# Fused attention, routed experts and mixer: the weighing of two heads in two column halves, and the seam before the mixer

## What is computed

```python
# attention, for each batch and head
q_d, k_d, v_d = means over groups of 4 positions          # 144 positions
out_up    = repeat(softmax(q_d @ k_d.T / 8) @ v_d, 4)
out_local = softmax(mask(q @ k.T / 8)) @ v                # mask: |i - j| < 4
x = out_up + out_local
# experts: one of 8 per position (w1: 512 x 1024, w2: 1024 x 512)
y[b, s] = p[e] * (relu(x[b, s] @ w1[e]) @ w2[e])
# mixer
u   = y + (relu(y.T @ w_tok1) @ w_tok2).T
out = u + relu(u @ w_ch1) @ w_ch2
```

## Time and profile before

| | us |
|---|---|
| median of 3 runs | 924.77 (924.2 to 925.93) |
| the profiled execution, own time | 922.74 |
| its span, as the trace has it | 921.1 |
| mean granted TensorE clock in it | 0.981 of full |

### The profile page before, as it was taken

How to read it: one execution, slowest core, us unless ns; L and a number is a source line. 1 busy time by engine, 2 the same in 40 slices (tenths; PEclk the granted TensorE clock), 3 DMA queues, 4 the chain that set the end, 5 groups by cost and what they waited for, 6 DMA issues and landing times.

```text
span 921.1 us, 13441 instructions
## 1 busy us (share of the span) xinstructions
PE 866.1 (94%) x4511; PEld 719.9 (78%) x4512; DVE 441.6 (48%) x893; ACT 348.8 (38%) x876; POOL 233.2 (25%) x355
## 2 busy tenths in 40 slices
PE   6888989889899999999999959999999999999998
PEld 4676767657478888888878847999999889999997
DVE  5786978878663462435663547312122353121211
ACT  4666775655253352435562433111111121111110
POOL 6886876774322212221212210000000000000000
PEclk9899999999799999999999989999999999999999
DMA  9558776630162842346652532002010010000000
GB/s 160 110 101 204 152 140 139 148 129 12 52 214 73 281 167 94 119 148 219 211 181 79 194 95 99 1 1 69 1 55 15 7 62 1 1 35 1 35 1 35
DMA packets 94128, 88.44 MB, mean 96 GB/s; under 512 B 63213, under 2 KB 68991, under 8 KB 94079
## 3 DMA queue, kind: packets, MB, share of 16 engines
q1 hardware_dynamic: 90203, 75.21, 29.8%
q0 software_dynamic: 3840, 12.59, 4.1%
q10 hardware_dynamic: 36, 0.01, 0.0%
HBM read 72.31 MB, written 15.48 MB: 95 GB/s over the span
## 4 chain that ended last, share of the span: by engine, by line
PE 75%; DVE 8%; POOL 7%; issue 4%; DMA 3%; ACT 2%; SPq 1%; POOLq 0%; ACTq 0%; DVEq 0%
PE bank L1648 16%; PE bank L1650 16%; PE bank L1649 16%; PE bank L1700 4%; PE bank L1707 4%; PE bank L1701 4%; PE bank L1691 2%; POOL asb L735 2%; PE bank L1525 2%; DMA stage<-in_moe_w 1%; PE bank L1478 1%; PE bank L1572 1%; PE bank L1656 1%; DVE aT L1121 1%; POOL ptmp L721 1%
## 5 line engine op out<-in xcount | busy, mean ns | idle before, releaser
L1371 DVE SCALAR_TENSOR_TENSOR h2l<-bank,h2h 128x384 fp32r<-128x384 f32 x72 | 40.1, 558 | 190.0 <-ACT h2h L1022 190.0
L1022 ACT ACTIVATE h2h<-bank 128x384 fp32r<-128x384 f32 x72 | 35.4, 492 | 229.7 <-PE bank L1650 229.7
L1648 PE MATMUL bank<-uTh,W 128*128 128x384 f32 x288 | 98.1, 340 | 0.0
L1649 PE MATMUL bank<-uTl,W 128*128 128x384 f32 x288 | 97.5, 338 | 0.0
L1650 PE MATMUL bank<-uTh,W 128*128 128x384 f32 x288 | 97.1, 337 | 0.0
L1650 PE MATMUL bank<-W,h2l 128*128 128x512 f32 x216 | 84.5, 391 | 0.0
L1648 PE MATMUL bank<-W,h2h 128*128 128x512 f32 x216 | 84.3, 390 | 0.0
L1649 PE MATMUL bank<-W,h2h 128*128 128x512 f32 x216 | 84.1, 389 | 0.0
L1309 DVE TENSOR_TENSOR W<-stage,W 128x1024 fp32r<-128x1024 f32 x56 | 66.7, 1220 | 21.2 <-ACT W L968 18.7
L1700 PE MATMUL bank<-W,hTh 128*128 128x512 f32 x184 | 76.3, 415 | 0.0
L968 ACT ACTIVATE W<-stage 128x1024 fp32r<-128x1024 f32 x56 | 58.0, 1055 | 45.2 <-DVE ysb L1327 24.3
(11 more groups left out here) (224 smaller groups left out, 1804.6 us busy)
## 6 DMA issues: line engine op xcount, KB each, us to landing
stage<-in_moe_w SPq DMA_DIRECT2D x56, 512.0 KB, 4.6
vl<-in_v SPq DMA_DIRECT2D x40, 128.0 KB, 3.7
qraw<-in_q SPq DMA_DIRECT2D x32, 144.0 KB, 4.9
kraw<-in_k SPq DMA_DIRECT2D x32, 144.0 KB, 5.3
v<-in_v SPq DMA_DIRECT2D x8, 576.0 KB
ub<-y_dr SPq DMA_DIRECT2D x18, 256.0 KB, 4.5
out<-ob SPq DMA_DIRECT2D x18, 256.0 KB, 2.1
x_dr<-xrow SPq DMA_DIRECT2D x16, 256.0 KB, 3.3
```

Of the source, the lines that this page charges most:

```text
L1022: act.activation(dst, bank[bk][:, 0:width], ACT.Relu).then_inc(relu_hi, 1)
L1371: dve.scalar_tensor_tensor(dst, bank[bk][:, 0:width], 0.0, hi.bitcast(F32), ALU.max, ALU.subtract).then_inc(bank_free, 1)
L1648: pe.matmul(ps, ah, bh, start=first, stop=False)
L1649: pe.matmul(ps, ah, bl, start=False, stop=False)
```

## The change

It has two parts.

1. `weigh` issues a pair's two heads as two matmuls, each with a stationary operand of 64 columns and the probabilities of one head alone. The first writes partitions 0 to 63 of the bank, the second 64 to 127, over the same columns. So the sums of a unit lie on 128 partitions in half as many columns, and `attended` takes them in one DVE instruction in place of two. `scores` is left as it is.
2. At the seam, the scaling in place (L1381), its wait and its semaphore go. `u_rows` reads the unscaled tile and multiplies by the share as it adds. PE gets `keep_busy(36, bank[3])` after the transpose L1740, ahead of its wait for `moe_done`.

```diff
             def attended(n):
                 if u < NDS:
                     pr, j = u // NPQ, u % NPQ
-                    for h in range(2):
-                        rows = slice(h * D, (h + 1) * D)
-                        last = dve.tensor_scalar_mul(odT[rows, hb % 2, pr, j * PQ:(j + 1) * PQ],
-                                                     ps_o[n % 2][rows, h * PQ:(h + 1) * PQ], 1.0 / POOLF)
+                    dve.tensor_scalar_mul(odT[:, hb % 2, pr, j * PQ:(j + 1) * PQ], ps_o[n % 2][:, 0:PQ], 1.0 / POOLF
+                                          ).then_inc(x_done, 1)
                 else:
...
-                    for h in range(2):
-                        rows = slice(h * D, (h + 1) * D)
-                        o = ps_o[n % 2][rows, 0:4 * lq].rearrange("d (r h n f) -> d r h n f", r=HP, h=2, f=POOLF)
-                        x = xT[rows, hb % 2 * HP:hb % 2 * HP + HP, Q0[t]:Q0[t] + lq].rearrange(
-                            "d r (n f) -> d r n f", f=POOLF)
-                        up = odT[rows, hb % 2, :, Q0[t] // POOLF:Q0[t] // POOLF + n4]
-                        last = dve.tensor_tensor(x, o[:, :, h], bc(up.unsqueeze(3), [D, HP, n4, POOLF]), ALU.add)
-                last.then_inc(x_done, 1)
+                    o = ps_o[n % 2][:, 0:HP * lq].rearrange("d (r n f) -> d r n f", r=HP, f=POOLF)
+                    x = xT[:, hb % 2 * HP:hb % 2 * HP + HP, Q0[t]:Q0[t] + lq].rearrange("d r (n f) -> d r n f", f=POOLF)
+                    up = odT[:, hb % 2, :, Q0[t] // POOLF:Q0[t] // POOLF + n4]
+                    dve.tensor_tensor(x, o, bc(up.unsqueeze(3), [P, HP, n4, POOLF]), ALU.add).then_inc(x_done, 1)
...
             def x_lo_tile(pr, i):
                 dve.scalar_tensor_tensor(xl[:, cols], ub[:, i, :], share, xh[:, cols].bitcast(F32), ALU.mult,
                                          ALU.subtract).then_inc(xl_done, 1)
-                dve.wait_ge(xl_done, 9 * pr + i + 1)
-                dve.tensor_scalar_mul(ub[:, i, :], ub[:, i, :], share).then_inc(xf_done, 1)
...
             def u_rows(pr, hb):
-                dve.wait_ge(xf_done, 9 * pr + (9 if hb else NK5))
+                dve.wait_ge(xl_done, 9 * pr + (9 if hb else NK5))
...
-                    tt(ub[rows, i, :], bank[2 + kk][rows, :], ub[rows, i, :], ALU.add).then_inc(bank_free, 1)
+                    dve.scalar_tensor_tensor(ub[rows, i, :], ub[rows, i, :], prob[rows, 9 * pr + i:9 * pr + i + 1],
+                                             bank[2 + kk][rows, :], ALU.mult, ALU.add).then_inc(bank_free, 1)
...
             def weigh(n):
+                heads = [slice(h * D, (h + 1) * D) for h in range(2)]
...
                     for kt in range(NPQ):
-                        mm = pe.matmul(ps_o[n % 2][:, 0:2 * PQ], vd[:, hb % 2, kt, pr * P:(pr + 1) * P],
-                                       aT[0:PQ, n % 2, kt * 2 * PQ:(kt + 1) * 2 * PQ], start=(kt == 0),
-                                       stop=(kt == NPQ - 1))
+                        for h in range(2):
+                            c = pr * P + h * D
+                            mm = pe.matmul(ps_o[n % 2][heads[h], 0:PQ], vd[:, hb % 2, kt, c:c + D],
+                                           aT[0:PQ, n % 2, (2 * kt + h) * PQ:(2 * kt + h + 1) * PQ], start=(kt == 0),
+                                           stop=(kt == NPQ - 1))
...
                     for pr in range(HP):
-                        cols = slice(pr * 2 * lq, (pr + 1) * 2 * lq)
-                        mm = pe.matmul(ps_o[n % 2][:, cols], vl[:, hb % 2, t, pr * P:(pr + 1) * P],
-                                       aT[:, n % 2, cols], start=True, stop=True)
+                        for h in range(2):
+                            c = pr * P + h * D
+                            mm = pe.matmul(ps_o[n % 2][heads[h], pr * lq:(pr + 1) * lq], vl[:, hb % 2, t, c:c + D],
+                                           aT[:, n % 2, (HP * pr + h) * lq:(HP * pr + h + 1) * lq], start=True, stop=True)
...
             pe.transpose(bank[7][:, 0:NT], probT[:, :], ident[0:NT, 0:NT]).then_inc(prob_turned, 1)
+            keep_busy(36, bank[3])
             pe.wait_ge(moe_done, 1)
```

More of the change, by code:

```diff
@@ L446, in build @@
         xh_done, xl_done = sem("xh_done"), sem("xl_done")
-        xf_done = sem("xf_done")
         bank_full = sem("bank_full")
```

## The result

The change takes **920.10 us** (median of 5 runs, 916.91 to 922.08) against 924.77 (5 runs, 923.34 to 925.93): a ratio of 0.9947, 95% interval 0.9922 to 0.9971. Predicted were 916.6 with a range of 911.5 to 922.5. So 4.7 us of an expected 8.2 came. The profiled execution is the median one: 920.10 its own time, 918.4 the span, 2.7 less than before.

A forecast was written before the change was run, and what follows sets the result against it. PE, busy 94%, bounds the kernel, with DVE or POOL setting the pace in stretches of attention. 5.7 + 2.6 + 1.6 - 1.7 = 8.2 us off 922.74 gives 914.5, as a median 916.6; range 911.5 to 922.5.

The forecast's parts named there:

- rival 2: Weighing on PE: the halves don't overlap and gain nothing; 5.6 us off, 919.2; chance 0.17.
- rival 4: Weighing: two drains a unit at 0.09 us, seen after a 10-column operand; 921.1 with overlap, 923.7 without; chance 0.10.
- A: Attended step in attention: two DVE instructions become one, saving 5.7 us on the chain, POOL limiting blocks 3 and 5.
- B: Weighing on PE: halves overlap partly, five slots for eight, shape change free; 2.6 us off, ends 0 and 5.9.
- rival 1: Attention: the weighing's halves overlap fully and the clock holds; 13.2 us off, 911.6; chance 0.12.
- C: Seam before the mixer: without the scaling, and with 36 matmuls for full clock, the last tile starts sooner; 1.6 us off.
- D: Granted clock in attention: one more half-clock stretch as PE has less work; costs 1.7 us.
- Others take over (3): Blocks 2, 4 and 6: ACT ends close behind; half of A and all of B go; 922.0; chance 0.13.
- Slower (5): Weighing: a drain at every change of half, no overlap; 5.7 us slower, 930.5; chance 0.08.

The follow-up runs named there:

- experiment 3: The change's seam without its 36 matmuls, attention as in the kernel before: 923.48 us, 0.9989 of the kernel before.
- the repeat: Under D and Sum, the change run again on another chip: 918.88 us, 0.9928; beside 912.57, the first hold kernel run again on another chip: 915.15 us, 0.9877.
- experiment 4: The change, but each head keeps its own columns and DVE its two instructions: 923.45 us, 0.9986 of the kernel before.
- experiment 5: As experiment 4, with both heads' operands in the same half of the array: 923.8 us, 0.9995 of the kernel before.
- the first hold kernel: The change plus 56 unused bfloat16 matmuls where blocks join, to hold the clock: 912.57 us, 0.9881 of the kernel before.
- experiment 2: The change's seam alone, weighing and attended step as in the kernel before: 922.07 us, 0.9979 of the kernel before.

## Why the prediction was right, and where it was not

Faster was right and the time lay in the range; the forecast was 3.5 us too low. The time alone does not bear the forecast out: 920.10 lies nearer to rival 2 (919.2) and rival 4 (921.1). What decides between them are the traces, term by term.

**A, the attended step (forecast 5.7):** right, 6.3 at equal clock. Where it lies was less exact: block 7, with no POOL behind it, gave 2.8 of it. In blocks 3 and 5 POOL took over, as the step said. From the fourth normalization of block 3 to the first of block 4 it is 16.2 us before and after, POOL's own pace.

**B, the weighing (2.6):** 1.5 in the profiles, nothing by medians, and two steps of it were wrong in opposite directions. The order of the passes does not limit the overlap to five slots: the records go in four pairs, so the halves overlap fully, as rival 1 had it. And the sentence that a change of the operand's shape costs nothing failed: it costs 0.09 us on entering and 0.09 on leaving, rival 4's two drains at the price of the 10-column row, and some 0.05 more in the first slot and in the matmul behind. Four slots are 0.41 us for the old 0.82; the switches and what follows them take back 0.29, so a local unit keeps 0.12 where 0.20 was forecast, and a pooled one nothing. That B came out as near as it did is in part luck, one error covering the other. The transposes' switch in the earlier trace rows stays the exception, with no loss on leaving a 64-column operand; no run shows why. The rule of the Trainium skill ("TensorEngine Tiling (Array Packing)", Key Properties: a change of mode drains the engine, different tiles work in parallel) thus bears out in both parts for the weighing, the drain with 0.09 us at each end.

**C, the seam (1.6):** 1.7 in the profile of the seam alone. The 36 matmuls ran at full clock (7.94 us) and brought the pace that they were for; that 0.7 us hangs on them is not shown (experiment 3). In the change's own profile only 1.1, since the tiles came later; the chain shows it:
```profile
547.76 5.17 DMA ub<-y_dr
552.95 0.73 ACT xh L1025
553.71 0.76 DVE xl L1371
554.51 0.50 PE bank L1644
```
The fifth tile starts at 554.51, 4.1 us after the first at 550.37, not 3.5: once DVE is quick enough, the load is what the last tile waits for.

**D, the clock (-1.7):** of the four terms this one missed by most. The mechanism was named, but "one more such stretch" was too few: four more in this profile, two more in the repeat. At half clock the kernel before loses 207.4 - 204.3 = 3.1 us in attention, the change 203.4 - 196.5 = 6.9. D was -3.8 in this profile. In the repeat's, with 201.0 us of attention, it is -1.4, so its size changes from one execution to the next. I had looked at the one join that stood nearest to the fall (1.85 of 3.4 us busy) and not at the others. A faster DVE makes every round end earlier, and the wait for POOL at the join longer, so PE was down to 0.76 and 0.93. That the merged instruction and not the shorter weighing does it rests on the counts under experiment 4. The prediction had named many new half-clock stretches in attention as a sign of being wrong altogether. They came, and the time stayed in the range because A held.

**Sum** for the profiled executions: 6.3 + 1.5 + 1.1 - 3.8 = 5.1. The experts took back 2.0 and the start 0.5, which leaves 2.6 of the 2.7 that the spans show. By medians, which average over that, it is 4.7 here and 7.1 in the repeat (918.88 against 925.99). With the forecast's D the sum would have been 7.2. In the profiled pair the 2.5 us of the experts and the start, of which the forecast says nothing, are a larger share of the shortfall than D's 2.1.

**The rivals.** Halves that do not overlap (2) fell with experiment 5 and the pairs. Others take over (3) is true from 94 to 103 and not elsewhere. Two drains (4) was right in its drains, and too low in its overlap. Slower (5) did not come: inside a unit no slot but the first is late. Full overlap (1) was right on the halves and wrong on the clock. Rival 1's time, 911.6, is nearly what the change with its clock held gives (912.57, and 915.15 in the repeat), by other terms: less from the halves, more from the clock.

## What to carry to other kernels

Two heads side by side on the partitions let one DVE instruction do the work of two at the price of one; that, not the matmuls, was the gain, and it counts where DVE is on the chain. Matmuls in two halves overlap fully, but each visit to that shape costs 0.09 us at either end, so short matmuls there give the gain back. An engine made faster ahead of a wait for a third engine lengthens PE's idle time at that wait: read PE's busy share just ahead of every join, not of the nearest one, and count what half clock costs behind it. A few unused matmuls there cost little when PE waits anyway: on this kernel they brought another 3.7 us side by side and 7.5 against the first measurement (1.2% below the kernel before in all), and on the kernel before 2.8, where blocks 2 and 4 grew by 0.4 us each.

## What the runs showed of the hardware

Two float32 matmuls of 64-column operands in different halves overlap fully, though the kernel issues the whole float32 matmul of one head ahead of the other's: their records start in pairs 5 to 7 ns apart, and eight of 120 columns take 0.56 us in two halves and 0.97 in one. Going from a wider operand to that shape costs 0.09 us, and going back 0.09 us and 0.04 to 0.06 in the matmul behind, in two halves as in one. In the chain the return shows as 0.14 us, at the mask (0.36 for 0.22) as at the pooled scores (0.64 for 0.50).

At the start of an execution the clock column can print 1.00 where no clock was recorded yet; the pace of like matmuls (0.43 us for 0.22) shows the half clock.

The time of one kernel varies from execution to execution, in part with the granted clock: the change's five runs go from 916.91 at a mean clock of 0.983 to 922.08 at 0.976. With the 56 matmuls the first hold kernel's six runs stand at 0.981 to 0.991, the slowest of them (915.99) at 0.981. The clock is not all of it: experiment 2's kernel took 922.69 us at 0.994 and 920.51 at 0.992, and the experts alone differ by 4.6 us between profiles. So a difference of 1 or 2 us between single profiles of this kernel says little; here the blocks of the attention were compared one by one instead.
